# A causal convolution inside a fused mixer: which engine adds the seven taps

## The reference

```python
# 1: dynamic convolution, H = 8 heads, K = 7 taps, 24 channels in a head
w = exp(weight_gen - max over K); w = w / (sum over K + 1e-9)
x_pad = x with K - 1 = 6 zero rows in front of the sequence
out[b, s, h, :] = sum over k of w[b, s, h, k] * x_pad[b, s + k, h, :]
# 2: u = out + real(fft over the sequence and the channels of out); layer norm, an MLP of width 768, residual
# 3: theta = x @ w_theta; y = w_tok_r @ (x cos theta) + w_tok_i @ (x sin theta);
#    u = x + y; u + relu(u @ w_ch)
```

## Time and profile before

| | |
|---|---|
| median of 3 runs | 3247.5 us (3244.93 to 3252.19) |
| profiled execution | 3247.57 us, its span 3245.6 us |
| busy in the span | PE 2981.7 us (92%), DVE 2596.3 (80%), POOL 1578.1 (49%), ACT 1299.9 (40%) |
| DMA | 618.36 MB, mean 191 GB/s |

### The profile page before, as it was taken

How to read it: one execution, slowest core, us unless ns; L and a number is a source line. 1 busy time by engine, 2 the same in 40 slices (tenths; PEclk the granted TensorE clock), 3 DMA queues, 4 the chain that set the end, 5 groups by cost and what they waited for, 6 DMA issues and landing times.

```text
span 3245.6 us, 57818 instructions
## 1 busy us (share of the span) xinstructions
PE 2981.7 (92%) x17218; PEld 2841.1 (88%) x17218; DVE 2596.3 (80%) x4304; ACT 1299.9 (40%) x2452; POOL 1578.1 (49%) x1527
## 2 busy tenths in 40 slices
PE   3555689999999799999999999999999999999999
PEld 3444459989898799999999999999999999999999
DVE  8999667777778887888878787887878788887776
ACT  1111236666666433433333333333333333333443
POOL 6666215666666653545445444544545354443221
PEclk8777899999999899999999999999999999999999
DMA  6676462232333465665656565565656656565442
GB/s 226 227 253 226 164 240 98 99 118 103 112 109 132 178 231 207 223 225 213 229 193 232 207 233 213 210 227 211 220 210 223 218 213 227 214 224 177 144 135 78
DMA packets 213452, 618.36 MB, mean 191 GB/s; under 512 B 20288, under 2 KB 61504, under 8 KB 211200
## 3 DMA queue, kind: packets, MB, share of 16 engines
q1 hardware_dynamic: 203600, 603.19, 52.3%
q10 hardware_dynamic: 9696, 13.37, 1.4%
HBM read 399.82 MB, written 216.66 MB: 190 GB/s over the span
## 4 chain that ended last, share of the span: by engine, by line
PE 76%; issue 7%; POOLq 6%; DVE 4%; DVEq 2%; ACT 2%; POOL 1%; DMA 1%; SPq 1%; ACTq 0%
PE banks L1576 56%; PE banks L1443 10%; POOLq L1047 5%; PE banks L1514 4%; PE banks L1516 2%; DVE zl L802 2%; PE banks L1500 2%; DVEq L850 1%; POOL head L1045 1%; ACT zh L1267 1%; PE banks L1655 1%; PE banks L1490 1%; PE banks L1492 1%; DMA m_scr<-mst 0%; DVE angle L790 0%
## 5 line engine op out<-in xcount | busy, mean ns | idle before, releaser
L1576 PE MATMUL banks<-zh,wh 128*128 128x384 f32 x3828 | 1294.5, 338 | 45.0 <-DVE rbuf L854 45.0
L1576 PE MATMUL banks<-zh,wl 128*128 128x384 f32 x3828 | 1281.5, 335 | 0.0
L1576 PE MATMUL banks<-zl,wh 128*128 128x384 f32 x3828 | 1280.9, 335 | 0.0
L854 DVE TENSOR_TENSOR rbuf<-rbuf,banks 128x384 f32<-128x384 f32 x1168 | 643.3, 551 | 251.6 <-PE banks L1576 217.5
L1576 PEld LDWEIGHTS banks<-zh,wh 128*128 128x128 f32 x3828 | 719.8, 188 | 67.1 <-DVE rbuf L854 47.4
L1576 PEld LDWEIGHTS banks<-zl,wh 128*128 128x128 f32 x3828 | 720.1, 188 | 0.0
L1576 PEld LDWEIGHTS banks<-zh,wl 128*128 128x128 f32 x3828 | 719.6, 188 | 0.0
L1079 POOL TENSOR_TENSOR wsum<-wraw 128x384 f32<-128x384 f32 x176 | 179.3, 1019 | 1106.3 <-DVE wl L797 980.8
L1259 ACT ACTIVATE wh<-wsum 128x384 fp32r<-128x384 f32 x704 | 370.2, 526 | 771.0 <-PE banks L1576 729.7
L797 DVE TENSOR_TENSOR wl<-wsum,wh 128x384 fp32r<-128x384 f32 x664 | 504.7, 760 | 39.4 <-ACT wh L1259 14.8
L1259 ACT ACTIVATE wh<-wraw 128x384 fp32r<-128x384 f32 x528 | 278.1, 527 | 497.0 <-PE banks L1576 497.0
(11 more groups left out here) (141 smaller groups left out, 4265.9 us busy)
## 6 DMA issues: line engine op xcount, KB each, us to landing
wraw<-w_pairs SPq DMA_DIRECT2D x176, 768.0 KB, 6.7
rbuf<-y_scr SPq DMA_DIRECT2D x176, 768.0 KB, 5.6
y_scr<-rbuf SPq DMA_DIRECT2D x160, 768.0 KB, 4.0
xin<-x_pad SPq DMA_DIRECT2D x22, 1728.0 KB, 8.2
z_scr<-zsc SPq DMA_DIRECT2D x33, 768.0 KB, 4.0
zraw<-z_scr SPq DMA_DIRECT2D x33, 768.0 KB, 7.4
x_scr<-x1s SPq DMA_DIRECT2D x22, 576.0 KB, 5.3
t_scr<-tst ACTq DMA_DIRECT2D x44, 288.0 KB, 8.0
```

What stands on the lines that cost most here:

```text
L854: dve.tensor_tensor(part, part, dst(k, i), ALU.add).then_inc(r_done, 1)
L1576: last = pe.matmul(dst, l[w][:, q, :], r[par][:, operand, q, :], start=starts and q == 0 and t == 0, stop=q == 2 and t == 2, skip_group_ch ...
```

## The change

The streams of all five engines change, all in the convolution stage.

- VectorE makes the same seven products, in another order (`TAP_ORDER`: 1, 2, 6, 3, 4, 5 in the first half, 1, 5, 2, 6, 3, 4 in the second), and adds nothing, but in the very last half. Each product of a tap now waits until the reader of the same tap buffer in the half before is done: for the additions of GpSimd that is `taps_added`, which now counts each addition, for TensorE's it is `tail_used`. The product into `head[h]` waits until TensorE has read the `head[h]` of the group before (`sum_ready`).
- GpSimd adds taps 1 to 5 in the first half and 1 to 4 in the second (`HEAD_TAPS`), two only in the last half.
- TensorE adds what is left (`TAIL_TAPS`: tap 6 in the first half, 5 and 6 in the second) and then `head[h]`, each as three products of 384 columns with the unit matrix, all accumulated in PSUM banks 3 to 5 (`sum_tail`, `sum_head`). The channel transform `dft_chan` goes to banks 0 to 2 for that, behind the sequence transform.
- ScalarE copies banks 3 to 5 into `x1s[h]` (`evac_x`) and tells SP and TensorE. Its order in a half is now `evac_x`, exponential, `evac_t`, `evac_a`.
- SP waits with `load_a` for the last product of the half, as before, now by the count of `tap_ready`.
- In the last half TensorE sums only `head` and one buffer, after VectorE has added four taps with three additions.

```diff
@@ -385,6 +385,26 @@
         def z_at(t, par, o, jj):
             return t[par][:, o, ds(jj, 1), :].rearrange("p o x -> p (o x)")
+        HEAD_TAPS = ((1, 2, 3, 4, 5), (1, 2, 3, 4))
+        TAIL_TAPS = ((6,), (5, 6))
+        TAP_ORDER = ((1, 2, 6, 3, 4, 5), (1, 5, 2, 6, 3, 4))
+        def final(g, h):
+            return isinstance(g, int) and (g, h) == (NG - 1, 1)
+        def head_taps(g, h):
+            return (1, 2) if final(g, h) else HEAD_TAPS[h]
+        def heads(g, h):
+            return 9 * g + 5 * h
+        def tails(g, h):
+            return 3 * g + h
         def four(t):
             return t[:].rearrange("p b j (h c) -> p b (j h) c", h=H)
@@ -410,7 +430,9 @@
         def _(sp):
             def load_a(g, h):
-                wait(sp, x_free, 2 * g + h - 1)
+                if g:
+                    sp.wait_ge(tap_ready, heads(g - 1, h) + len(HEAD_TAPS[h]))
                 for b in range(2):
                     sp.dma_start(win[h][:, 24 * b:24 * b + 24, :].rearrange("p (j h) k -> p j (h k)", j=3),
                                  wgen_v[:, 2 * h + b, ds(3 * g, 3), :]).then_inc(g_in[h], 16)
@@ -681,17 +703,29 @@
                 dve.tensor_tensor(soft_w(h), win[h][:], soft_sum(h).unsqueeze(2).broadcast_to([P, 48, K]), ALU.mult)
-            def weigh(h, k):
+            def weigh(g, h, k):
                 dst = tap[k - 1] if k else head[h]
-                return dve.tensor_tensor(four(dst), tap_x(h, k), tap_w(h, k), ALU.mult)
+                if not k:
+                    wait(dve, sum_ready, 2 * g + h - 1)
+                elif not (isinstance(g, int) and 2 * g + h == 0):
+                    bg, bh = (g, 0) if h else (g - 1, 1)
+                    if k in HEAD_TAPS[bh]:
+                        dve.wait_ge(taps_added, heads(bg, bh) + HEAD_TAPS[bh].index(k) + 1)
+                    else:
+                        dve.wait_ge(tail_used, tails(bg, bh) + TAIL_TAPS[bh].index(k) + 1)
+                made = dve.tensor_tensor(four(dst), tap_x(h, k), tap_w(h, k), ALU.mult)
+                if k in head_taps(g, h):
+                    made.then_inc(tap_ready, 1)
+                elif k and not final(g, h):
+                    made.then_inc(tail_ready, 1)
             def first_tap(g, h):
                 norm(g, h)
                 dve.drain()
                 dve.wait_ge(x_in[h], 16 * (g + 1))
-                weigh(h, 0)
+                weigh(g, h, 0)
             def convolve(g, h, following):
@@ -699,29 +733,23 @@
                     if following:
                         step(*following)
-                weigh(h, 1).then_inc(tap_ready, 1)
+                order = TAP_ORDER[h]
+                weigh(g, h, order[0])
                 soft(top_weight)
-                weigh(h, 2).then_inc(tap_ready, 1)
+                weigh(g, h, order[1])
                 dve.drain()
                 soft(shift)
-                weigh(h, 3).then_inc(tap_ready, 1)
-                weigh(h, 4).then_inc(tap_ready, 1)
+                weigh(g, h, order[2])
+                weigh(g, h, order[3])
                 soft(total)
-                weigh(h, 5)
+                weigh(g, h, order[4])
                 dve.drain()
                 soft(guard)
-                weigh(h, 6).then_inc(x_free, 1)
+                weigh(g, h, order[5])
                 dve.drain()
                 soft(inverse)
                 dve.drain()
                 soft(first_tap)
-                dve.wait_ge(taps_added, 2 * g + h + 1)
-                dve.tensor_tensor(tap[4][:], tap[4][:], tap[5][:], ALU.add)
-                dve.drain()
-                wait(dve, x1_out[h], 16 * g)
-                wait(dve, s_ready, 2 * g + h - 1)
-                dve.tensor_tensor(x1s[h][:].rearrange("p j (b d) -> p b j d", b=2), head[h][:], tap[4][:],
-                                  ALU.add).then_inc(x1_ready, 1)
             for step in (top_weight, shift, total, guard, inverse, first_tap):
                 step(0, 0)
@@ -733,10 +761,15 @@
                 convolve(g, 1, (g + 1, 0))
             convolve(NG - 1, 0, (NG - 1, 1))
             convolve(NG - 1, 1, None)
             dve.drain()
+            dve.tensor_tensor(tap[4][:], tap[4][:], tap[5][:], ALU.add)
+            dve.tensor_tensor(tap[2][:], tap[2][:], tap[3][:], ALU.add)
+            dve.drain()
+            dve.tensor_tensor(tap[4][:], tap[4][:], tap[2][:], ALU.add).then_inc(tail_ready, 1)
+            dve.wait_ge(sum_ready, 2 * NG)
             for s in range(4):
                 if s == 2:
                     dve.wait_ge(t_ready, 2 * NG)
@@ -1040,18 +1073,19 @@
         def _(pool):
             def taps(g, h):
-                for k in range(1, 5):
-                    pool.wait_ge(tap_ready, 4 * (2 * g + h) + k)
-                    last = pool.tensor_tensor(head[h][:], head[h][:], tap[k - 1][:], ALU.add)
-                    if k < 4:
+                for n, k in enumerate(head_taps(g, h)):
+                    pool.wait_ge(tap_ready, heads(g, h) + n + 1)
+                    pool.tensor_tensor(head[h][:], head[h][:], tap[k - 1][:], ALU.add).then_inc(taps_added, 1)
+                    if k != head_taps(g, h)[-1]:
                         pool.drain()
-                last.then_inc(taps_added, 1)
             for h in range(2):
                 taps(0, h)
-            with pool.Fori(1, NG) as g:
+            with pool.Fori(1, NG - 1) as g:
                 for h in range(2):
                     taps(g, h)
+            for h in range(2):
+                taps(NG - 1, h)
             pool.wait_ge(cwh_ready, 7)
@@ -1161,16 +1195,22 @@
                 act.wait_ge(w_shift, 2 * g + h + 1)
                 act.activation(win[h][:], win[h][:], ACT.Exp).then_inc(w_exp, 1)
+            def evac_x(g, h):
+                act.wait_ge(sum_ready, 2 * g + h + 1)
+                wait(act, x1_out[h], 16 * g)
+                act.activation(x1s[h][:], banks[:, 3:6, 0:2 * D], ACT.Copy).then_inc(x1_ready, 1)
             def evac_a(g, h):
                 act.wait_ge(s_ready, 2 * g + h + 1)
                 act.activation(a1[h][:], banks[:, 0:3, 0:3 * P], ACT.Copy).then_inc(a_ready, 1)
-            def evac_t(g, h):
+            def evac_t(g, h, first=0):
                 act.wait_ge(t_ready, 2 * g + h + 1)
                 wait(act, t_out[h], 32 * g)
-                act.activation(tst[h][:].rearrange("p j b d -> p j (b d)"), banks[:, 3:6, 0:2 * D],
+                act.activation(tst[h][:].rearrange("p j b d -> p j (b d)"), banks[:, first:first + 3, 0:2 * D],
                                ACT.Copy).then_inc(t_evac, 1)
                 act.drain()
                 for w in range(2):
@@ -1180,20 +1220,26 @@
             def step_a(g, first=False, more=True):
                 for h in range(2):
+                    evac_x(g, h)
                     if more:
                         exps(g + 1, h)
-                    evac_a(g, h)
                     if h:
                         evac_t(g, 0)
                     elif not first:
                         evac_t(g - 1, 1)
+                    evac_a(g, h)
             exps(0, 0)
             exps(0, 1)
             step_a(0, first=True)
             with act.Fori(1, NG - 1) as g:
                 step_a(g)
-            step_a(NG - 1, more=False)
+            evac_x(NG - 1, 0)
+            evac_t(NG - 2, 1)
+            evac_a(NG - 1, 0)
+            evac_x(NG - 1, 1)
+            evac_a(NG - 1, 1)
+            evac_t(NG - 1, 0, 3)
             evac_t(NG - 1, 1)
@@ -1210,7 +1256,6 @@
                 for s in range(4):
                     group_b(j, s)
-            act.wait_ge(x1_ready, 2 * NG)
             act.wait_ge(cw_in, 112)
             for hi, raw in ((w1h[:], w1_raw[:, 0]), (w1s[0:D2], w1_raw[0:D2, 1]), (w1t[D2:P], w1_raw[D2:P, 1]),
                             (w2s[:, :, 0], w2_raw[:]),
@@ -1444,40 +1489,79 @@
                 return last
+            def add_part(part, j, start, stop):
+                return pe.matmul(bank[3 + j][:, 0:2 * D], idn[:], part[:, :, j, :], start=start, stop=stop)
+            def sum_tail(g, h):
+                wait(pe, x1_ready, 2 * g + h)
+                for n, k in enumerate(TAIL_TAPS[h]):
+                    pe.wait_ge(tail_ready, tails(g, h) + n + 1)
+                    for j in range(3):
+                        last = add_part(tap[k - 1], j, n == 0, False)
+                    last.then_inc(tail_used, 1)
+            def sum_head(g, h):
+                pe.wait_ge(taps_added, heads(g, h) + len(HEAD_TAPS[h]))
+                for j in range(3):
+                    last = add_part(head[h], j, False, True)
+                last.then_inc(sum_ready, 1)
             def dft_seq(g, h):
                 q = 2 * g + h
                 pe.wait_ge(x1_ready, q + 1)
-                wait(pe, a_ready, q)
+                if final(g, h):
+                    pe.wait_ge(a_ready, q)
+                else:
+                    wait(pe, t_evac, q)
                 for j in range(3):
```

(33 more changed lines are left out.)

## The result

| | before | after |
|---|---|---|
| median | 3247.48 us (3244.93 to 3252.19) | 3199.99 us (3197.93 to 3200.73) |
| profiled execution, its span | 3247.57, 3245.6 | 3200.73, 3198.9 |
| mean granted clock of the span | 0.968 | 0.988 |

The ratio is 0.9851, with a 95% interval of 0.9834 to 0.9868: 47.5 us faster. Forecast were 3209 us and a range of 3195 to 3224.

A forecast was written before the change was run, and what follows sets the result against it. VectorE bounds the convolution stage; after the change GpSimd does, at 27.2 us a pair. First T at 25.7, ten periods to 297.7, tail to 324.1 instead of 362.16: 3247.57 - 38.1 = 3209 us, range 3195 to 3224.

The forecast's parts named there:

- Who is late next: Convolution stage, per pair of halves: GpSimd's own work of 25.2 us exceeds VectorE's 23.8, so GpSimd is late next.
- The two stalls: GpSimd's second half of a pair: 0.45 us lost to `tap2`, 1.4 to `tap3`, making the period 27.2 us.
- The clock at the head of the pair: TensorE idles 3.9 us, then starts each pair's head sum at half clock, 0.05 to 3.9; period 27.2 us.
- the lower end: Period of a pair if TensorE did not start it at half clock: 25.9 us instead of 27.2.
- TensorE's price: Three unit-matrix products of one tap, 1152 columns: 1.95 us at full clock, 3.8 at half.
- The start: First group: GpSimd's fifth addition, whose end is T, ends at 25.7 us for g = 0.
- The tail: Last group of the convolution stage: last `evac_t` at T + 26.35 = 324.1 us, where before it started at 362.16.
- rival 1: TensorE's clock does not fall between pairs: period 25.9 us, tail 24.5, total 3195 us; chance 0.15.
- The same distances: Behind the convolution stage: what follows hangs on the last `evac_t` at unchanged distances, everything shifted by 38 us.
- Rival 2: `win` weights land late and hold VectorE, then GpSimd: period 30 to 31 us, total 3238 to 3248; chance 0.06.
- Rival 3: TensorE does not return to full clock: its 42.8 us a pair bind, total about 3380 us; chance 0.04.
- Rival 4: Each wait in a pair is a few tenths longer: 28.5 us a pair, total 3222 us; chance 0.13.

The follow-up runs named there:

- e8: Changed kernel with ScalarE's exponential before `evac_x`, `win` loaded early, tap 2 before tap 5 in the second half, still nine GpSimd additions a pair: 3183.16 us.
- e6: Changed kernel with eight GpSimd additions a pair, ScalarE's exponential before `evac_x`, and `win` loaded about half a pair sooner: 3172.53 us, ratio 0.9766.
- e1: Changed kernel with ScalarE making the next group's exponential before `evac_x` instead of behind it: 3189.73 us, ratio 0.9819.
- e2: Changed kernel with four more TensorE products with a zero matrix behind the last sequence transform of each pair: 3190.11 us, ratio 0.9821.
- e4: Changed kernel with ScalarE's exponential before `evac_x` and second-half taps ordered 1, 2, 5, 6, 3, 4: 3186.03 us, ratio 0.9804.
- e7: Changed kernel with only the early load of the softmax weights `win` added: 3201.88 us, against 3201.97 for the changed kernel in the same group.
- e3: Changed kernel with the first half's fifth addition moved from GpSimd to TensorE, so GpSimd adds eight in a pair: 3179.18 us, ratio 0.9788.
- e5: Changed kernel with eight GpSimd additions a pair and ScalarE's exponential before `evac_x`: 3181.91 us, ratio 0.9798.

## Why the prediction was right, and where its sizes were off

- **Who is late next: GpSimd.** Right. Its own work of 25.2 us was measured clean in e8 (25.14). VectorE's 23.8 came out as 24.1 in e6.
- **The two stalls.** The forecast's gaps before the second and the third addition were 0.65 and 1.6 us (0.45 and 1.4 lost, and the usual 0.20). The rows have 0.74, and 1.34 in a pair at half clock. Right in place and cause; e1 took the second away through ScalarE's queue, e2 through the clock, e4 the first through the order of the taps.
- **The clock at the head of the pair.** Right in eight pairs of ten; the rule that a loop pays for the way up in every pass, by which the prediction took 27.2 for all, did not hold in the other two. The term that was mis-sized is the period: 27.2 in every pair, where ten pairs average 26.63. That is 5.7 us of the 9, and it has two parts. Two pairs began at the full clock: 2.2 us. The other eight average 26.85 and not 27.2, which makes 3.5 us over ten: in the pair shown TensorE enters the head sum at the full clock, which falls half a microsecond into it, where the forecast had it at half clock from the start; the sums of the eight pairs take 3.3 to 3.9 us, in the pair shown `tap3` is ready at T + 7.25 and not at 7.5, and GpSimd's gap before that addition is 1.29 us on average instead of 1.6. The forecast had 3.9 us of idle time before each head sum; behind a steady pair at half clock it is 3.1 to 3.7, behind the two at the full clock 4.1 and 3.9, since TensorE then has its work done sooner. That the clock would fall in most pairs was right by a narrow margin: idle times of 3.2 us held it and 3.5 us did not, and in e4 the same 3.44 us did either. The prediction named 25.9 as the lower end, and that is what e1 and e2 show when the clock or its way is cured.
- **TensorE's price.** Three unit-matrix products at the full clock were put at 1.95 us, worked out from the columns of the second transform. Measured: 1.94 from one such group to the product behind it (98.40 to 100.34 us).
- **The start.** T of g = 0 came at 25.2 instead of 25.7 us: 0.5.
- **The tail.** Forecast T + 26.35. Measured 318.00 - 291.5 = 26.5, with the head sum at half clock (3.88 us); in e1 and e2, at the full clock, it is 24.8, where rival 1 has 24.5.
- **Behind the stage.** "The same distances" held to 2.5 us, the scatter shown above. The profiled execution was 0.7 us above its median. With the 5.7, 0.5 and 2.5 this makes 9.4, less 0.15 of the tail: the 9 us.
- **Rival 2, late weights.** Refused for this kernel: 0.7 us of waits in the stretch, and e7 gains nothing. It has its place once GpSimd is relieved (9.3 us of waits in e3, and 9 us of the time between e5 and e6).
- **Rival 3, TensorE stays at half clock.** Refused: the clock was back at 1.00 some 4 us after the start of the head sum.
- **Rival 4, many small waits.** Refused: the gaps are 0.22 and not 0.20, about 0.15 us in a pair.

What the prediction did not price at all is the choice inside the change. It took nine additions on GpSimd as given and found that they make it the bound; that 23.8 of VectorE stood below 25.2 of GpSimd was the sign that the ninth was put on the wrong engine. It costs 21 us as the kernel stands, about half of it by way of the clock, and 11 to 12 where the other waits are cured (e8 against e6).

## What to carry to other kernels

When a change relieves the engine at the limit, work out the period of every engine that receives something, one by one: the smallest maximum is the goal, and an operation that makes its new owner the slowest belongs elsewhere. Where engines work in order of their text, follow a late start through the queues: some 1.6 us more on TensorE (3.75 instead of 2.20) reached GpSimd by way of two instructions on ScalarE that had nothing to do with each other, and swapping these two was worth as much as keeping the clock up. A wait that costs nothing today (e7) can be the next limit tomorrow (e6), so try such edits together with the one that uncovers them.

## What was not expected of the hardware

- Eight recorded products with a zero matrix, 2.75 us in a pair, made the kernel 10 us faster, since the granted clock stayed at 1.00 (e2).
- At the same place in the program the clock fell in some pairs and held in others, after idle times of 3.47 and 3.08 us. The same instructions gave pairs of both kinds in one execution, and in e4 even after the same idle time, 3.44 us.
- The loads of `xin` and the stores of `x1s` did not get slower when the stage moved its bytes in less time. The share of DMA rose from 0.67 to 0.78, yet `xin` landed in 8.3 us (8.2 before), and the stores of `x1s` in 3.0 (5.3 before). Only the small loads of `win` took longer, 2.5 us (2.0 before):

```profile
xin<-x_pad SPq DMA_DIRECT2D x22, 1728.0 KB, 8.3
```
